# Keys loaded, transposed and placed as whole rows, with new order tables, in an attention and feed-forward kernel

## The reference

```python
q_pool = q.reshape(B, H, S // 2, 2, D).mean(axis=3)        # (4, 8, 576, 64)
scores = np.matmul(q_pool, k.transpose(0, 1, 3, 2)) / np.sqrt(D)
attn = softmax(scores)                                     # over 1152 keys
x = np.matmul(attn, v)                                     # -> x, 2304 x 512
g = curve(x @ w_in); y = g @ w_out                         # 512 -> 2048 -> 512
out = max(y @ w1, y @ w2, y @ w3) @ w2_out                 # 512 -> 768 -> 512
```

## Time and profile before

| | |
|---|---|
| median of 3 runs | 1243.48 us (1241.06 to 1243.55) |
| the profiled execution | 1244.4 us, of it 1242.7 us span |
| attention | from the start to about 534 us |
| feed-forward | from there to 1242.7 us, 709 us |
| TensorE / VectorE / ScalarE busy in the span | 98% / 59% / 50% |

### The profile page before, as it was taken

How to read it: one execution, slowest core, us unless ns; L and a number is a source line. 1 busy time by engine, 2 the same in 40 slices (tenths; PEclk the granted TensorE clock), 3 DMA queues, 4 the chain that set the end, 5 groups by cost and what they waited for, 6 DMA issues and landing times.

```text
span 1242.7 us, 19281 instructions
## 1 busy us (share of the span) xinstructions
PE 1223.2 (98%) x7061; PEld 1074.9 (87%) x7061; DVE 732.5 (59%) x1508; ACT 618.2 (50%) x1433; POOL 274.7 (22%) x240
## 2 busy tenths in 40 slices
PE   7999999999999999999999999999999999999998
PEld 6999999999999999878888888888898878787887
DVE  5999999999999999853443443443452132212222
ACT  5898899889988998832222222222331111112011
POOL 3133333333333333379000000000192000000000
PEclk8999999999999999999999999999999999999999
DMA  3565656666666664434100000000041010101010
GB/s 95 96 114 114 116 115 116 116 115 116 116 115 115 113 116 79 78 98 143 30 1 1 1 1 1 1 1 1 2 136 33 1 34 1 35 1 35 1 35 17
DMA packets 124604, 76.17 MB, mean 61 GB/s; under 512 B 62560, under 2 KB 111712, under 8 KB 124512
## 3 DMA queue, kind: packets, MB, share of 16 engines
q1 hardware_dynamic: 124512, 74.94, 29.8%
HBM read 47.71 MB, written 4.79 MB: 42 GB/s over the span
## 4 chain that ended last, share of the span: by engine, by line
PE 94%; DVE 2%; ACT 2%; issue 0%; SPq 0%; DMA 0%; POOL 0%; DVEq 0%; ACTq 0%
PE hid L936 34%; PE acc L962 16%; PE values L519 12%; PE trans L437 11%; PE scores L502 7%; PE scores L503 6%; PE acc L994 5%; PE trans L457 1%; PE trans L447 1%; DVE neg_max_parts L649 1%; DVE pT_lo L663 1%; ACT probs L568 1%; ACT qT L1027 0%; ACT pT_hi L559 0%; DVE qT L1033 0%
## 5 line engine op out<-in xcount | busy, mean ns | idle before, releaser
L936 PE MATMUL hid<-qT,w_slots 128*128 128x512 f32 (+1 forms) x1680 | 367.8, 372 | 0.0
L936 PEld LDWEIGHTS hid<-qT,w_slots 128*128 128x128 f32 x1680 | 293.6, 188 | 61.2
L649 DVE TENSOR_REDUCE neg_max_parts<-scores 128x1 f32<-128x384 f32 x432 | 227.1, 550 | 8.9 <-PE scores L503 4.3
L663 DVE TENSOR_TENSOR pT_lo<-trans,pT_hi 128x384 fp32r<-128x384 f32 x432 | 225.7, 546 | 5.0 <-ACT pT_hi L559 4.4
L559 ACT ACTIVATE pT_hi<-trans 128x384 fp32r<-128x384 f32 x432 | 205.8, 494 | 42.0 <-PE trans L437 38.8
L568 ACT ACTIVATE probs<-scores,neg_max 128x768 f32<-128x768 f32 (+1 forms) x288 | 212.5, 742 | 6.5 <-DVE neg_max L656 5.6
L437 PE MATMUL trans<-ident,probs 128*128 128x128 f32 x1296 | 201.0, 275 | 4.9 <-DVE pT_lo L663 2.8
L502 PE MATMUL scores<-kT,qT 128*128 128x384 f32 x480 | 182.4, 380 | 2.0 <-ACT probs L568 1.5
L437 PEld LDWEIGHTS trans<-ident,probs 128*128 128x128 f32 x1296 | 155.9, 140 | 20.5 <-DVE pT_lo L663 8.9
L503 PE MATMUL scores<-kT,qT 128*128 128x384 f32 x480 | 162.6, 339 | 0.0
L1059 ACT ACTIVATE excess<-rise,halves 128x512 f32<-128x512 f32 (+1 forms) x80 | 54.5, 681 | 185.9 <-DVE rise L1129 185.9
(11 more groups left out here) (77 smaller groups left out, 1494.2 us busy)
## 6 DMA issues: line engine op xcount, KB each, us to landing
kT<-k_split SPq DMA_DIRECT2D x60, 288.0 KB, 5.4
k_raw<-in_k SPq DMA_DIRECT2D x32, 288.0 KB, 6.1
v_raw<-in_v SPq DMA_DIRECT2D x32, 288.0 KB
q_raw<-in_q SPq DMA_DIRECT2D x32, 256.0 KB, 3.2
k_split<-value_all SPq DMA_DIRECT2D x64, 72.0 KB, 2.9
out<-X SPq DMA_DIRECT2D x18, 256.0 KB, 2.9
q_raw<-in_moe_w_out SPq DMA_DIRECT2D x14, 256.0 KB, 3.1
k_raw<-in_moe_w SPq DMA_DIRECT2D x12, 256.0 KB, 3.2
```

Of the source, the lines that this page charges most:

```text
L649: dve.tensor_reduce(neg_max_parts[:, par, n:n + 1], scores[:, score_banks(s)[n], 0:SB], AX_X, ALU.max, negate=True).then_inc(parts_done, 1)
L663: dve.tensor_tensor(*tile_places(pT[1], src, s % TILES, g), hi.bitcast(F32), ALU.subtract).then_inc(p_lo_done, 1)
L936: last = pe.matmul(out_bank, weight(slot, part, half, k), x[:, k, cols], start=(k == 0 and part == 0 and x is x_hi), stop=(k == KC - 1 and ...
```

## The change

Keys keep whole rows. `load_k` is one transfer for both heads, with runs of 9 x 64 floats, where it was two with runs of 64. A 128-column block to be transposed is now two neighbouring keys of one head (the middle one is the last key of head 0 and the first of head 1). So the transposed odd keys and even keys lie on different partition halves, and `place_k` takes six transfers, one of 1152 columns and one each of 512 and 640 for either split part. The keys of a tile stand in the order 1, 3, 5, 7, 0, 2, 4, 6, 8 (`KEY_BLOCKS`), and the products with the values pick `v_split` in that order. The number of instructions on TensorE, ScalarE, VectorE and GpSimd is the same. The three tables are new.

```diff
-S1.2 S1.0 K0
-T0.0 W2:10-14 S2.0 T0.1 W2:14-16 T0.2 S2.1 W2:16-18 S2.2 K1 S3.0 W3:0-9
+S1.2 S1.0 S2.0
+T0.0 W2:10-13 T0.1 W2:13-16 K0 W2:16-18 S2.1 S2.2 T0.2 W3:0-8 S3.0
...
-    k_raw = shared["k_raw"][:].rearrange("p (t h d) -> p t h d", t=KT, h=2)
+    k_raw = shared["k_raw"][:].rearrange("p (h t d) -> p h t d", h=2, t=KT)
+    KEY_BLOCKS = [*range(1, KT, 2), *range(0, KT, 2)]
+    ODD = KT // 2 * P
...
         def load_k(pair):
-            for h in range(2):
-                src = k_heads[bass.ds(head(pair) + h, 1)].rearrange("h p (t d) -> p (h t) d", d=D)
-                sp.dma_start(k_raw[:, :, h, :], src).then_inc(k_loaded, 16)
+            src = k_pairs[bass.ds(head(pair) // 2, 1)].rearrange("c p h n -> p (c h) n")
+            sp.dma_start(k_raw.rearrange("p h t d -> p h (t d)"), src).then_inc(k_loaded, 16)
...
-            for h in range(2):
-                for a in range(2):
-                    copy_parts(sp, kT[rows_of(a), pair % 2, h, :], k_parts[rows_of(h), a, :], k_placed)
+            places = kT[:, pair % 2].rearrange("p h s -> p (h s)")
+            for a in range(2):
+                copy_parts(sp, places[rows_of(a), ODD:ODD + S], k_parts[rows_of(0), a, :], k_placed)
+                copy_parts(sp, places[rows_of(a), 0:ODD], k_parts[rows_of(1), a, 0:ODD], k_placed)
+                copy_parts(sp, places[rows_of(a), ODD + S:2 * S], k_parts[rows_of(1), a, ODD:S], k_placed)
...
             for j in range(GK):
-                src = k_raw[:, g * GK + j].rearrange("p h d -> p (h d)")
+                src = rows[:, (g * GK + j) * P:(g * GK + j + 1) * P]
```

More of the change, by code:

```diff
@@ L40 @@
 PE_ORDER = """
-S1.2 S1.0 K0
-T0.0 W2:10-14 S2.0 T0.1 W2:14-16 T0.2 S2.1 W2:16-18 S2.2 K1 S3.0 W3:0-9
[L43 to L50, removed]
+S1.2 S1.0 S2.0
+T0.0 W2:10-13 T0.1 W2:13-16 K0 W2:16-18 S2.1 S2.2 T0.2 W3:0-8 S3.0
+T1.0 W3:8-9 S3.1 S3.2 T1.1 T1.2 W3:9-12 S4.1 W3:12-13
+T2.0 T2.1 S4.2 T2.2 S4.0 K1 K2 W3:13-16 S5.0 W3:16-17
+T3.0 W3:17-18 T3.1 T3.2 S5.1 S5.2 S6.0 Q0 V0:0-6
+T4.0 V0:6-8 T4.1 V0:8-9 S6.1 S6.2 Q1 T4.2 V0:9-15 S7.1
+T5.0 V0:15-17 S7.2 Q2 T5.1 V0:17-18 S7.0 S8.0 T5.2 V1:0-6
+T6.0 T6.1 V1:6-9 S8.1 S8.2 T6.2
+T7.0 V1:9-12 S9.0 V1:12-15 T7.1 V1:15-17 T7.2 V1:17-18 S9.1 S9.2
+T8.0 T8.1 V2:0-3 S10.1 V2:3-9 T8.2 V2:9-10
 """
 ACT_ORDER = """
[L53 to L61, removed]
+H0.0 E1.0 H0.1 W2 K0 E1.1 H0.2 E2.0
+H1.0 E2.1 H1.1 H1.2 E3.0
+H2.0 E3.1 H2.1 H2.2 K1 K2 E4.0
+H3.0 E4.1 W3 H3.1 H3.2 Q0 E5.0
+H4.0 E5.1 H4.1 Q1 H4.2 E6.0
+H5.0 E6.1 H5.1 V0 Q2 H5.2 E7.0
+H6.0 E7.1 H6.1 H6.2
+H7.0 E8.0 H7.1 H7.2 V1 E8.1
 H8.0 H8.1 E9.0 E9.1 H8.2
@@ L64 @@
 DVE_ORDER = """
[L65 to L74, removed]
+R M2.0
+L0.0 M2.1 M2.2 L0.1 K0 L0.2 M3.0 M3.1 M3.2
+L1.0 L1.1 M4.1 L1.2
+L2.0 M4.2 L2.1 M4.0 L2.2 K1 K2 M5.0
+L3.0 M5.1 M5.2 L3.1 L3.2 Q0 M6.0
+L4.0 M6.1 M6.2 L4.1 Q1 L4.2 M7.1
+L5.0 M7.2 M7.0 Q2 L5.1 M8.0 L5.2
+L6.0 M8.1 M8.2 L6.1 L6.2
+L7.0 M9.0 L7.1 M9.1 M9.2 L7.2
+L8.0 M10.1 L8.1 M10.2 M10.0 L8.2
 """
@@ L104, in attention_phase @@
     assert D == 64 and 2 * TAIL == P and PAIRS % 2 == 0 and B == 4
-    k_heads = k.rearrange("b h (p t) d -> (b h) p (t d)", t=KT)
+    k_pairs = k.rearrange("b (c h) (p t) d -> (b c) p h (t d)", h=2, t=KT)
     v_heads = v.rearrange("b h (p t) d -> (b h) p (t d)", t=KT)
@@ L443, in key_transposes @@
             wait_bank(group)
-            pe.wait_ge(k_loaded, 32 * (pair + 1))
+            pe.wait_ge(k_loaded, 16 * (pair + 1))
+            rows = k_raw.rearrange("p h t d -> p (h t d)")
             for j in range(GK):
-                src = k_raw[:, g * GK + j].rearrange("p h d -> p (h d)")
+                src = rows[:, (g * GK + j) * P:(g * GK + j + 1) * P]
                 last = pe.transpose(trans[:, BANK[group], j * P:(j + 1) * P], src, ident[:])
@@ L467, in first_transposes @@
                 for j in range(GK):
-                    src = first_split[:, g * GK + j].bitcast(F32).rearrange("p a d -> p (a d)")
+                    h, block = (g * GK + j) // KT, (g * GK + j) % KT
+                    src = first_split[:, h * KT + KEY_BLOCKS[block]].bitcast(F32).rearrange("p a d -> p (a d)")
                     last = pe.transpose(trans[:, bank, j * P:(j + 1) * P], src, ident[:])
@@ L481, in tile_scores @@
             if first and t == 0 and pair > 0:
-                pe.wait_ge(k_placed, 64 * pair)
+                pe.wait_ge(k_placed, 96 * pair)
                 pe.wait_ge(q_lo_done, pair * QG)
@@ L518, in value_products @@
                     pe.wait_ge((p_hi_done, p_lo_done)[part], (pair * TILES + t + 1) * GROUPS)
-                last = pe.matmul(values[:, 0:HALF], v_split[:, h, kt].rearrange("p a d -> p (a d)"),
+                last = pe.matmul(values[:, 0:HALF], v_split[:, h, KEY_BLOCKS[kt]].rearrange("p a d -> p (a d)"),
                                  pT[part][:, h, kt, half * HALF:(half + 1) * HALF],
@@ L718, in dve_program @@
             part = first_split[:, h * KT:(h + 1) * KT]
-            raw = k_raw[:, :, h, :]
-            dve.wait_ge(k_loaded, 32)
+            raw = k_raw[:, h]
+            dve.wait_ge(k_loaded, 16)
             dve.tensor_copy(part[:, :, 0, :], raw).then_inc(first_split_done, 1)
@@ L749, in attention_phase @@
     ends = dict(scores_done=(scores_done, ALL_TILES * GROUPS),
-                keys_placed=(k_placed, 64 * (PAIRS - 1)),
+                keys_placed=(k_placed, 96 * (PAIRS - 1)),
                 k_raw_free=(k_trans_done, (PAIRS - 1) * KG), q_raw_free=(q_trans_done, (PAIRS - 1) * QG),
```

## The result

| | before | changed |
|---|---|---|
| median | 1243.51 us of 12 runs | 1245.57 us of 12 runs |
| ratio, 95% interval | | 1.002 [1.001, 1.0029] |
| the profiled execution | 1244.4 us | 1245.01 us |
| of it span | 1242.7 us | 1243.3 us |

What follows compares the result with a forecast made beforehand. TensorE and VectorE were taken to bound an undisturbed pair, with at most 0.3 us to spare in 31.4. Terms -0.7 - 4.0 + 0.5 + 0.5 = -3.7 us took the profiled 1244.4 to 1240.7, forecast as 1240; range 1235.5 to 1246.5.

Steps and rivals of the forecast that it cites:

- The start: Before the first scores: one key issue and whole key rows save 0.7 us, bounds 0 and 1.3.
- rival D: Clock at the start: keys landing earlier avoid the fall to half clock, 1.5 to 2 us less, 1238; chance 0.06.
- The period at K2: K1 and K2 behind H2.2 on ScalarE: cushion grows from 0.4 to about 0.95 us, hiding late starts, -4.0 us.
- VectorE's own order: VectorE in each pair: wait at M2.1 and banks up to 0.3 us late cost 0 to 4.5 us, taken as 0.5.
- The floor of 31.4: Undisturbed attention pair: TensorE is busy throughout, so no order table can bring it much below 31.4 us.
- V0 to V1: ScalarE's copy of V0 ahead of V1: cushion falls from 0.64 to 0.09 us, cost 0 to 3, taken as 0.5.
- The transfers: Six key placements: extra issues hide behind the transfers, V1's copy gains cushion to 0.8 to 1.2 us, cost nothing.
- Rival C: Six transfers hold up value half 3 and so V1's copy; TensorE loses 0.8 us in 14 pairs, 1251; chance 0.06.
- rival A: No difference: late H2.2 strikes elsewhere and small waits eat the start's gain; 1241 to 1245, centre 1243; chance 0.27.
- rival B: VectorE or V0's copy binds each pair: 0.4 us lost in 15 pairs, late H2.2 half hidden, 1246; chance 0.11.

Runs made afterwards that it cites:

- e6: Changed kernel with TensorE's S2.1 and S2.2 moved ahead of K0: 1253.09 us, ratio 1.0073 to the kernel before.
- e3: Changed kernel with VectorE's L0.1 moved ahead of M2.1 and M2.2: 1252.4 us, ratio 1.0046 to the kernel before.
- e12: Changed kernel with the old tables for the period's start and tiles 0 to 3, new ones for tiles 4 to 8: 1250.65 us, ratio 1.0054.
- e9: Kernel before, with exponentials from pair 1 on leaving out the last 64 columns of a group: 1245.74 us, ratio 0.9993.
- e8: Changed kernel, with exponentials from pair 1 on leaving out the last 64 columns of a group: 1246.58 us, ratio 1.0 to the kernel before.
- e1: Changed kernel with the three order tables of before: 1243.97 us, ratio 0.9982 to the kernel before.
- e2: Kernel before, old transfers kept, with the three new order tables: 1249.41 us, ratio 1.0027.

## Why the prediction was wrong, step by step

**The start, -0.7.** Right in kind, a little small: the queries land 1.0 us earlier. By the Trainium skill's page "DMA: Bandwidth & Descriptors" (section Specifications) the estimate had been 1.5 us; the measured 1.0 is nearer to the rows' 0.8 than to it. (How the 1.5 came about isn't said; the keys' 0.59 MB once more at the rows' 281 GB/s would be an estimate of 2.1 us.) The further 1.5 us of the profile is the clock's for 0.9 to 1.1 (rival D had this case, at 1.5 to 2 us) and the tables' for 0.4. Most of the clock's part was given back in pair 0, where the clock fell instead.

**The period at K2, -4.0.** About -2.7 in this profile, and not by the mechanism of the step. I had assumed that the delays keep coming and that a larger cushion hides all but 0.7 of 5.4 us. They went with the key groups, came in two pairs only, and cost 0.8 and 1.1 us for 0.6 and 1.0 us late: nothing was hidden. In the other profiles with the new tables at this place ScalarE is over 0.3 us late at the key groups in none to six pairs, and pairs 1 to 14 are together 0.8 (e6) to 6.0 us (e3) over their undisturbed length; with the old tables it is 3.3 (e12) to 8.1 us (e9). So the gain has the forecast's sign, and how large it comes out in one profile is luck. Nor was the old cushion 0.4: in pair 10 of the kernel before H2.2 is 0.35 us later than in pair 9, and the pair is 0.32 longer.

**VectorE's own order, +0.5.** This is the step that failed. I walked the tables, found the wait at M2.1 and banks up to 0.3 us late, gave it 0 to 4.5 us, and took 0.5 "since the old order lives on equally thin cushions". It measured 0.27 x 14 = 3.8 us, near the upper bound. The reason that I gave was no evidence. The old order had the thin cushions at its places and its 31.44 already contained what they cost, 0.52 us by the starts; the new order's cost 0.84. The step also counts 30.8 us of VectorE's work where the reading of the rows had 31.1; with that and the wait of 0.4 it comes to 31.5, over the 31.44. Nor were the walk's places the right ones: T6.1, its worst, is not late at all, and S7.2 and T4.0, 0.14 and 0.13 us late, it does not name. And it wasn't VectorE's order alone: e3, e6 and e8 show the loop through ScalarE's exponentials, which I had not walked.

**The floor of 31.4.** I took TensorE's 31.44 busy of 31.44 for its own work and said that no order could come much below. A matmul's record includes short waits: the old order with lighter maxima takes 31.15 and the new one with both engines lighter 31.20, with the same matmuls.

**Pair 0.** No step spoke of it, and it costs 1.7 us by e1 and e2, of which up to 0.8 is the clock's. The new order leans on W2 and W3 between its groups, which the first pair doesn't have; that this is why S2.1 waits 1.93 us is read from the tables and not tested.

**V0 to V1, +0.5.** No wait was found at V1 in the pair read; the cushion is 0.18 us. The 0.5 was not spent.

**The transfers, 0.** Right. Half 3 comes earlier than before, no copy of V1 waits, and the tables of before with the new transfers are 0.18% faster. Six placements are issued in 4.61 us, and the pair has no wait for them. Rival C does occur, with the other tables: half 3 is 0.5 to 1.8 us late for V1's copy in three pairs of e1, and TensorE waits for it.

By cases, the median of 1245.57 lies between rival A's range (1241 to 1245) and rival B's 1246. The mechanism is B's: 0.27 us lost in each pair where it had 0.4, and about half of the late starts' cost gone (2.7 of 5.4). I had given it 0.11, and its argument against, again the old order's cushions, was the same error.

**What stays open.** Shown: the 0.27 us is the tables'; it isn't VectorE's load alone, nor the wait at M2.1; it is made at five places in both halves of the period, less what three others no longer lose; S3.1, T4.0 and most of S7.2 go when the other two engines are lighter. Not shown: whether the late starts at T3.2 and S7.0, which stay, are waits for the other engines at all, and which loop would have to be shortened to get the 0.27 us back. Also open is the cause of ScalarE's late starts around the key groups; they appeared with either order.
